# A delta-rule attention and two expert layers on one core: two small steps of the row scaling moved in the engines' order, and one wait added

## What is computed

```python
for t in range(S):
    kt, vt, bt = (k_n[:, :, t], v[:, :, t], beta[:, :, t, None])
    y[:, :, t] = np.einsum('bhd,bhde->bhe', q[:, :, t], state)
    v_old = np.einsum('bhde,bhd->bhe', state, kt)
    state = state + bt[:, :, :, None] * np.einsum('bhd,bhe->bhde', kt, vt - v_old)
```

## Time and profile before

| | |
|---|---|
| median of three runs | 1038.01 us |
| the profiled execution, whole | 1034.28 us |
| its span | 1032.5 us |
| PE busy | 904.3 us (88%) |
| DVE busy | 654.0 us (63%) |
| ACT busy | 482.5 us (47%) |
| POOL busy | 299.8 us (29%) |

### The profile page before, as it was taken

The page is one execution under the profiler, slowest core; times in us unless marked ns, Lnnn a source line. Parts: engine busy times, 40 slices in busy tenths (PEclk is TensorE's granted clock), DMA queues, the critical chain, the costliest instruction groups (busy, mean ns, idle before and its releaser), DMA issues.

```text
span 1032.5 us, 29294 instructions
## 1 busy us (share of the span) xinstructions
PE 904.3 (88%) x10418; PEld 672.1 (65%) x10418; DVE 654.0 (63%) x1579; ACT 482.5 (47%) x1080; POOL 299.8 (29%) x773
## 2 busy tenths in 40 slices
PE   3348889889788898839899999999999999999998
PEld 2237879778687787728777777776645454545544
DVE  5337787779878787658997988966752434233221
ACT  3124556567656755515845737544533232323212
POOL 4754556786868863410000000001101010100000
PEclk9999999999999999959999999999999999999999
DMA  6467575556443344039626638387501010101000
GB/s 162 77 175 180 122 185 127 123 143 134 92 87 74 88 85 110 33 128 313 239 83 216 244 123 269 132 240 273 186 1 62 1 62 1 62 15 46 15 16 31
DMA packets 214806, 122.70 MB, mean 119 GB/s; under 512 B 161648, under 2 KB 199536, under 8 KB 214672
## 3 DMA queue, kind: packets, MB, share of 16 engines
q1 hardware_dynamic: 136368, 68.41, 23.2%
q10 hardware_dynamic: 75232, 43.07, 15.5%
q0 software_dynamic: 3072, 9.44, 2.9%
HBM read 69.63 MB, written 26.87 MB: 93 GB/s over the span
## 4 chain that ended last, share of the span: by engine, by line
PE 44%; POOL 14%; DVE 13%; issue 9%; SPq 7%; DMA 5%; DVEq 4%; ACT 2%; another core or an unknown queue 0%; ACTq 0%; POOLq 0%
PE psum L1665 20%; PE psum L1684 7%; POOL arena L720 4%; POOL arena L717 4%; PE psum L1600 4%; DMA arena<-blocks 3%; SPq L650 3%; SPq L631 3%; PE psum L1613 3%; DVE arena L1249 2%; DVE arena L1168 2%; DVE arena L1261 2%; DVE arena L1239 2%; DVEq L1254 1%; DVEq L1246 1%
## 5 line engine op out<-in xcount | busy, mean ns | idle before, releaser
L1665 PE MATMUL psum<-arena 128*128 128x512 f16 x972 | 212.4, 379 | 0.4 <-DVE arena L1312 0.4
L1665 PEld LDWEIGHTS psum<-arena 128*128 128x128 f16 x972 | 95.0, 98 | 112.5 <-DVE arena L1312 0.8
L791 POOL DMA_INDIRECT arena<-y_sorted,arena x24 | 23.0, 959 | 456.2 <-DMA y_sorted<-arena 249.2
L1600 PE MATMUL psum<-arena 128*128 128x128 f16 x2232 | 147.8, 221 | 8.1 <-DVE arena L1249 3.4
L1600 PEld LDWEIGHTS psum<-arena 128*128 128x128 f16 x2232 | 134.3, 99 | 28.3 <-issue 8.7
L1613 PE MATMUL psum<-arena 128*128 x744 | 142.4, 327 | 4.5 <-DVE arena L1239 4.3
L1358 DVE SCALAR_TENSOR_TENSOR arena<-psum,arena 128x512 f32<-128x512 f32 x36 | 27.0, 751 | 141.7 <-PE psum L1665 141.7
L856 ACT ACTIVATE arena<-psum 128x256 f16<-128x256 f32 x144 | 52.2, 380 | 101.4 <-PE psum L1445 96.3
L1613 PEld LDWEIGHTS psum<-arena 128*128 128x128 f16 x744 | 68.5, 98 | 38.0 <-issue 7.1
L979 ACT ACTIVATE arena<-psum 128x256 f16<-128x256 f32 x124 | 47.3, 381 | 88.8 <-PE psum L1600 84.4
L1168 DVE SCALAR_TENSOR_TENSOR arena<-arena 128x384 f16<-128x384 f32 x128 | 74.5, 624 | 3.7 <-ACT arena L815 3.4
(11 more groups left out here) (233 smaller groups left out, 1835.7 us busy)
## 6 DMA issues: line engine op xcount, KB each, us to landing
arena<-arena SPq DMA_DIRECT2D x62, 384.0 KB, 3.3
arena<-in_moe_w_dram ACTq DMA_DIRECT2D x57, 384.0 KB, 4.1
arena<-inverses SPq DMA_DIRECT2D x24, 512.0 KB, 5.2
arena<-in_moe_w_dram SPq DMA_DIRECT2D x16, 384.0 KB, 4.3
y_sorted<-arena ACTq DMA_DIRECT2D x31, 192.0 KB, 3.7
x_sorted<-arena SPq DMA_DIRECT2D x7, 768.0 KB, 6.1
arena<-in_k_dram SPq DMA_DIRECT2D x24, 192.0 KB, 3.4
arena<-in_v_dram ACTq DMA_DIRECT2D x24, 192.0 KB, 3.3
```

Of the source, the lines that this page charges most:

```text
L1600: last = nc.tensor.matmul(psum[:, n % 2, fc * P:fc * P + P], w1[:, at:at + P], xT16[:, s, y, kc * P:kc * P + P], start=(i == 0), stop=(i = ...
L1665: last = nc.tensor.matmul(psum[:, 2 + 3 * (f % 2) + m, :], up_weight(w, m, kc, f), x16[:, par, kc, x, :], start=(i == 0), stop=(i == len(t ...
```

## The change

Three edits, none of which alters what is computed: in ACT's list W moves from behind p40 to behind "root", ahead of p61; in DVE's list "scale rows" moves from behind L, with ahead -4, to behind E0 at the beginning of a slot, with ahead -5; and DVE's step S waits for `y_mm` (PE's Y2 of the same tile) as well as for `s_mm`.

```diff
             "ACT": [("square", 3), ("p50", -4), ("p41", -4), ("q", -3), ("Tk", 1), ("Tq", -4), ("p60", -4), ("N0", 0),
-                    ("cum", -6), ("p51", -4), ("last0", -4), ("root", 3), ("p61", -4), ("N1", 0), ("weigh", -8), ("split", -6), ("p40", -3),
-                    ("W", -6), ("Y", -5), ("V", -5), ("last1", -4), ("X", -5), ("v", -2)],
-            "DVE": [("U", -4), ("E0", -3), ("K1", 2), ("K0", 2), ("S", -4), ("M40", -2), ("Q0", -3), ("Q1", -3), ("E1", -3),
-                    ("inverse", 4), ("L", -4), ("scale rows", -4), ("M50", -2), ("M41", -2), ("C0", -3), ("C1", -3), ("B", -3), ("sum", 5),
+                    ("cum", -6), ("p51", -4), ("last0", -4), ("root", 3), ("W", -6), ("p61", -4), ("N1", 0), ("weigh", -8), ("split", -6), ("p40", -3),
+                    ("Y", -5), ("V", -5), ("last1", -4), ("X", -5), ("v", -2)],
+            "DVE": [("U", -4), ("E0", -3), ("scale rows", -5), ("K1", 2), ("K0", 2), ("S", -4), ("M40", -2), ("Q0", -3), ("Q1", -3), ("E1", -3),
+                    ("inverse", 4), ("L", -4), ("M50", -2), ("M41", -2), ("C0", -3), ("C1", -3), ("B", -3), ("sum", 5),
...
                 if what == "S":

                     dve.wait_ge(s_mm, t + 1)
+                    dve.wait_ge(y_mm, t + 1)
```

## The result

The changed kernel takes 1047.69 us (median of 11 runs, 1042.19 to 1054.4), the kernel before 1038.01 us (median of 11 runs beside it). The ratio is 1.0105 with a 95% interval of 1.0076 to 1.0135: slower by about 10 us, where 1046 was forecast. The profiled execution took 1047.62 us with a span of 1045.8 us, 13.3 longer than before; the medians differ by 9.7.

What follows compares the result with a forecast made beforehand. In attention, POOL's eliminations were taken to bound long stretches, PE with DVE and ACT short ones. Terms 0 + 3.6 + 2.0 + 0.6 + 2.2 = 8.4 us on the median 1038.01 gave 1046.4, predicted as 1046, range 1037 to 1056.

Steps and rivals of the forecast that it cites:

- The meeting of W and its scale: ACT's W waits for DVE's "scale rows" until about 1.6 us after U's start, in every stretch.
- The price in one stretch: In tile 9 KQ starts about +5.6 us after U instead of +3.60; the stretch grows by 2.0 us.
- Term 1: Tiles 1 to 8: short stretches grow, but PE's waits for the inverses or U take it in; 0 us.
- already late at 231.65: Sign of being wrong: tiles 1 to 8 have already lost time at 231.65 us, U of tile 9.
- Term 2: Tiles 9 to 16: later KQ costs 9.6 us after DVE's gain, PE's waits absorb up to 6.05; 3.6 us.
- Term 3: Tiles 18 to 22, with "split" only or nothing: KQ at +4.6 against +3.72; 2.0 us, bounds 0 and 4.
- term 4: DVE's S waits for Y2, making M40 up to 0.1 late in tiles 18 to 22; 0.6 us, bounds 0 and 4.2.
- Term 5: PE's added idle times in attention bring two more falls to the low clock; 2.2 us, bounds 0 and 8.8.
- The rival with a fall in each stretch: PE idles twice in each loaded stretch, so its clock falls each time: 15 us, so 1053; chance 0.08.
- Cover: POOL's elimination and norm hide ACT's late N1 at no cost; without them, up to 3 us in a pair of stretches.
- Everything is paid: POOL's chain moves with PE, so PE's waits in attention absorb nothing: 16 us, so 1054; chance 0.10.
- Gain on DVE: Taking "scale rows" from between L and M50 saves 0.25 us a stretch, bounds 0 and 0.27.

Runs made afterwards that it cites:

- E0: Not a run: a step of DVE's list, right behind U at the beginning of a slot; no measured time of its own.
- e2: Changed kernel with W put back behind p40, scale rows and S's wait as changed: 1.0006 of the kernel before.
- e3: Changed kernel with scale rows put back behind L, W still ahead of p61 and S's wait kept: 0.9985 of the kernel before.
- e6: Changed kernel with W one place later on ACT, behind p61: 1.0115 of the kernel before.
- e7: Changed kernel with W behind split, ahead of p40: 1.0038 of the kernel before.
- e9: The changed kernel measured again, unaltered, on another chip: 1.0103 of the kernel before.
- e10: Changed kernel without S's wait for Y2, measured a second time, beside the changed kernel: 1.0102 of the kernel before.
- e1: Changed kernel without S's wait for Y2, first measurement: 1.0077 of the kernel before.
- e8: Kernel before with only W moved, to behind root and ahead of p61: 0.9994 of the kernel before.
- e12: Kernel before with DVE's step "scale", which waits for POOL's norm, moved from a slot's end to behind E0 of the next: 1.0023 of the kernel before.
- e5: Changed kernel with scale rows later still on DVE, behind K0 and ahead of S: 1.0506 of the kernel before.

## Why the prediction was right, step by step

- **The meeting of W and its scale.** Right in place and size: 22 waits of L892 for L1079, W at +1.56 (predicted +1.6), p61 at +2.1 (+2.2). The single wait was longer than the 2 to 5 us I had said, up to 7.2. e2 and e3 show that both moves are needed.
- **The price in one stretch.** KQ at +5.70 in tile 9 and +5.4 to +5.7 in tiles 10 to 16 (predicted +5.6), in tiles without weigh and split together, where nothing else holds it up, +4.4 (predicted +4.6). p40 was earlier than I had it, +4.7 instead of +4.9. e6 and e7 show that it is what stands between the wait and p40, N1, weigh and split, that makes it dear: p61 alone out of the queue (e6) saves nothing, all four out of it (e7) most.
- **Term 1, tiles 1 to 8: 0.** Measured +1.1 at U of tile 9, of which 0.6 were there at tile 0, ahead of any W. The shift rises to +3.6 at tile 4 and goes back to -0.3 at tile 8: the short stretches lose, and the waits for the inverses give it back. I had named "already late at 231.65" as a sign of being wrong; e9, e10 and e1 have +3.2, +2.5 and +3.3 there, but so has e8 (+3.2) without any loss. So the term is right within the 2 or 3 us by which single executions differ, and no better shown than that.
- **Term 2, tiles 9 to 17: 3.6.** Measured 5.9 - 1.1 = 4.8 from U of tile 9 to U of tile 17. Right within what one trace can tell (e9 has 7.3, e10 4.3). KQ's delays in tiles 9 to 16 add up to 10.9 us, in e9 and e10 too (predicted 11.6). The waits that were to take it in did so: from tile 9 to tile 17 those for U, without the one of tile 9, fell from 6.8 to 2.2 us, and those for L742 from 2.6 to nothing, 7.2 in all where I had 6.05. The steps of the shift are at tiles 10 and 14, the ends of the two stretches in which PE had no wait to lose, +2.1 and +2.3.
- **Term 3, tiles 18 to 22: 2.0, and term 4, 0.6.** This is the term that was mis-sized: from U of tile 18 to U of tile 23 the shift grows by 5.5, and by 5.1 both in e9 and in e10. KQ's delay makes 2.8 of it, 1.2 of them in tile 18. There the prediction misread the kernel: it has "split" only or nothing in tiles 18 to 22, but ACT runs both "weigh" and "split" in the stretch of tile 18, so that KQ comes at +5.58 and not at +4.6. The rest comes at the end of the stretches: U of tiles 19, 20 and 23 starts 1.0, 2.1 and 1.3 us behind the end of its matmuls (L1499), where it was 0.3, 0.3 and 0.6. What this is stays open, but W's wait does not explain it: e12, in which W waits for nothing in these tiles, has 1.9 us at U of tile 23 and 1.1 at U of tile 19, and e8, with one wait of W there (1.4 us), has 1.9 and 1.5. Nor does every execution have it: in e1, the kernel of e10, it is 0.3 and 0.04 us at U of tiles 20 and 23, and the shift grows by 1.7. It is not S's wait either, as e10 has it too. So of the 5.5 only KQ's 2.8 is shown to come from the change (e1, e9 and e10 have 2.7). Term 4 can't be told from 0, nor 0.6 from 0.
- **Term 5, the clock: 2.2.** In the changed kernel it was about 0. The profiled execution spent no more time at the low clock in attention than before, 17 us against 20; e9's trace has 31, so the median says more: over 12 runs that of the granted clock is 0.972, as in before's runs beside the siblings. This error hid the one of term 3, and that is luck. The rival with a fall in each stretch is what e5 does, not the change.
- **Cover.** From U of tile 1 to U of tile 23 POOL waits for ACT's N1 (L850) in neither trace, and its L748, which needs it, waits for PE alone, 10.6 us before and 11.0 after: ACT's late N1 cost POOL nothing, as said. "Everything is paid" is out: the waits of PE for inverses and L742 did shrink, by 8 us.
- **Gain on DVE.** -0.25 a stretch was in the sum, 2.0 us of it in term 2; no run tries it alone. e3 and e8, which differ from the changed kernel in it, show no loss without it. e2, which has it with W late, is at 1.0006, so no gain shows there, but there K's 0.25 us are paid (KQ +3.86 for +3.60). The gain stays unproven.

The sum was 8.4 us; the medians differ by 9.7. The place and the price of the wait were foreseen; that the total is off by only 1.3 us owes something to errors that cancel, the clock's 2.2 too much against what terms 2 and 3 lacked.

## What to carry to other kernels

A step moved in one engine's order is cheap or dear by where its producer stands in the other engine's order: write down for the moved pair when the one is made and when the other asks, in one clock (here U's start), before looking at any duration. The price of a wait is not its length but what is queued behind it and when that is needed: 57 us of waiting cost 0.24%, 85 us 1%, and with the two long steps and what comes before them put ahead of the wait, 15 us of it were left and a little over a third of the cost. And a wait that PE gets in every round should be kept short: here, with waits for ACT of 1 us, the clock stayed up, and with 2.5 to 3 us it did not.

## What was not expected of the hardware

With PE's waits for ACT of up to 1.1 us, two in a stretch, the median granted clock stayed at 0.972; with single ones of up to 1.9 us (e6) it was 0.964, and of up to 3.1 us (e5) 0.944. A reader who sees only one execution can be misled by this: the profile of e1 fell on an execution of 1047.78 us, 48 us of its attention at the low clock, when its median was 1041.74. Two chips also gave the same pair of kernels (without S's wait, and before) as 1.0077 and 1.0102, with intervals that overlap; within one kernel runs spread by 1%, so a part of 3 us can't be read from two measurements that were not made together.
